# A banded attention and MoE kernel: limits on ScalarE's queue, a shorter flag, values loaded ahead, bias tables in three column parts, identity products on TensorE

## The reference

```python
q, k, v: (2, 8, 768, 64);  n_global = 8;  n_local = 96
scores = (1 / sqrt(64)) * q @ k.T
rel = pos[:, None] - pos[None, :]
is_global = pos[None, :] < n_global
is_local = (rel >= 0) & (rel < n_local)
dist = where(is_global & ~is_local, n_local, abs(rel))
scores += -slopes[head] * dist                 # slopes = 2 ** (-(head + 1)), 8 heads
scores = where(is_global | is_local, scores, -1e9)
attn_out = softmax(scores) @ v
x = attn_out, as 1536 rows of 512
x = rmsnorm(x) * rms_g;  x = (silu(x @ w_gate) * (x @ w_val)) @ w_out
out = sum over the top 2 of 8 experts of weight * (relu(x @ w1[e]) @ w2[e])
```

## Time and profile before

| | |
|---|---|
| Median of 3 runs | 792.08 us (790.52 to 793.17) |
| The profiled execution | 793.64 us |
| Its span, first to last instruction | 791.9 us |
| TensorE busy | 770.3 us, 97% of the span |
| VectorE, ScalarE, GpSimd busy | 381.7, 321.3, 203.6 us |
| Mean granted clock of TensorE | 0.993 of full speed |

### The profile page before, as it was taken

One profiled execution on the slowest core, in us unless ns is written; L12 is line 12 of the kernel. 1 busy time (PEld: TensorE's weight loads), 2 busy tenths in 40 slices (PEclk: granted clock), 3 DMA queues, 4 the chain that ended last, 5 costly groups with the idle time before them and its releaser, 6 DMA issues.

```text
span 791.9 us, 11494 instructions
## 1 busy us (share of the span) xinstructions
PE 770.3 (97%) x4294; PEld 626.5 (79%) x4294; DVE 381.7 (48%) x723; ACT 321.3 (41%) x627; POOL 203.6 (26%) x273
## 2 busy tenths in 40 slices
PE   6999989999999999999999999999999999999994
PEld 4777667887878887878888987788898889898883
DVE  6777775553624235343245463535264454454331
ACT  4777874441334123351134632434243344443321
POOL 4568750000000300002300145141333423232311
PEclk9999999999999999999999999999999999999997
DMA  7868403510010000100313365336254365645221
GB/s 183 210 151 269 114 18 111 159 55 0 1 54 1 0 1 1 53 1 1 106 54 120 111 180 138 94 86 207 46 175 114 91 190 132 165 153 140 49 46 23
DMA packets 76378, 75.29 MB, mean 95 GB/s; under 512 B 46302, under 2 KB 53982, under 8 KB 76320
## 3 DMA queue, kind: packets, MB, share of 16 engines
q1 hardware_dynamic: 68560, 61.64, 26.4%
q0 software_dynamic: 7760, 12.89, 8.2%
HBM read 62.32 MB, written 13.75 MB: 96 GB/s over the span
## 4 chain that ended last, share of the span: by engine, by line
PE 92%; DVE 4%; issue 2%; ACT 1%; POOL 1%; DVEq 0%; POOLq 0%; ACTq 0%
PE banks L515 26%; PE banks L546 13%; PE banks L1048 11%; PE banks L1069 10%; PE banks L1111 8%; PE banks L1077 4%; PE banks L1090 4%; PE banks L1687 3%; PE banks L1722 3%; PE banks L1702 2%; PE banks L1657 2%; PE banks L1683 1%; PE banks L1039 1%; PE banks L1025 1%; PE banks L1086 1%
## 5 line engine op out<-in xcount | busy, mean ns | idle before, releaser
L515 PE MATMUL banks<-XN,W_mid 128*128 128x512 f32 x552 | 134.5, 396 | 0.0
L515 PEld LDWEIGHTS banks<-XN,W_mid 128*128 128x128 f32 x552 | 103.5, 188 | 25.5 <-issue 1.0
L406 POOL DMA_INDIRECT slots<-entry,slot_x x24 | 24.5, 1019 | 268.1 <-DVE slot_x L837 261.7
L1069 PE MATMUL banks<-W_mid,XN 128*128 128x512 f32 x240 | 72.2, 399 | 0.0
L515 PE MATMUL banks<-XN,W 128*128 128x512 f32 x288 | 70.5, 397 | 0.0
L515 PEld LDWEIGHTS banks<-XN,W 128*128 128x128 f32 x288 | 53.5, 188 | 14.3 <-issue 2.0
L652 ACT ACTIVATE HT<-act_b 128x512 fp32r<-128x512 f32 x36 | 22.8, 634 | 95.3 <-DVE act_b L758 87.2
L1602 POOL TENSOR_TENSOR prob<-prob,rinv 128x512 f32<-128x512 f32 (+1 forms) x47 | 46.8, 996 | 40.4 <-DVE rinv L1895 40.3
L1111 PE MATMUL banks<-W_mid,XN 128*128 128x512 f32 x180 | 56.6, 406 | 0.0
L756 DVE TENSOR_TENSOR act_b<-act_b,banks 128x512 f32<-128x512 f32 x36 | 24.7, 685 | 64.1 <-ACT act_b L645 56.8
L936 POOL DMA_INDIRECT out_dram<-xT x16 | 27.7, 1729 | 103.5 <-DVE xT L1250 98.2
(11 more groups left out here) (232 smaller groups left out, 1437.2 us busy)
## 6 DMA issues: line engine op xcount, KB each, us to landing
stage<-in_moe_w_dram SPq DMA_DIRECT2D x64, 512.0 KB
rawv<-in_v_dram SPq DMA_DIRECT2D x16, 192.0 KB, 3.1
out_dram<-zrow SPq DMA_DIRECT2D x1, 3072.0 KB, 12.6
moe_rows<-xT SPq DMA_DIRECT2D x12, 256.0 KB, 2.5
rawq<-in_q_dram SPq DMA_DIRECT2D x14, 192.0 KB, 3.1
rawk<-in_k_dram SPq DMA_DIRECT2D x14, 192.0 KB, 3.3
stage<-in_moe_w_gate_dram SPq DMA_DIRECT2D x4, 512.0 KB
stage<-in_moe_w_val_dram SPq DMA_DIRECT2D x4, 512.0 KB
```

Of the source, the lines that this page charges most:

```text
L515: last = nc.tensor.matmul(bank[2 * kind + n % 2][:], up_weight(kind, hw, k, c), xn[:, hx, k, :], start=(m == 0 and k == 0), stop=(m == 2 a ...
L1069: last = nc.tensor.matmul(bank[5 + t][:], he_pair[:, k, hh, t * P:(t + 1) * P], w2_part(e, hw, k), start=(q == 1), stop=(q == 24))
```

## The change

The two limits are loaded from ScalarE's queue, ahead of its table load, and no longer from SyncE's. SyncE loads the values of pair 0 right after the first halves of queries and keys, and makes the shifted values of pair 0 ahead of the loads of pair 1. VectorE reaches the flag by four operations behind the limits where there were six, all of the form with one scalar and two inputs. The tables are made in three column parts (128, 256, 256) with a semaphore for each, so that score 0, 1 and 2 wait for a part each. TensorE multiplies the identity by itself nine times ahead of the flag and twice ahead of score 0; nobody reads the result (bank 4). Preparations 2 and 3 of pair 0 stand behind score 2 in TensorE's order and behind the exponentials of unit 1 in ScalarE's, and each preparation of pair 1 is given one unit later (`prep_round`).

```diff
@@ sync
-            sp.dma_start(lims_i[:, 0, :], n_global.bitcast(I32).partition_broadcast(P)).then_inc(s_lim, 16)
-            sp.dma_start(lims_i[:, 1, :], n_local.bitcast(I32).partition_broadcast(P)).then_inc(s_lim, 16)
...
+            load_values(0)
             load_queries_keys(0)
-            load_values(0)
             for m in range(PAIRS):
+                if m == 0:
+                    shifted_values(m)
                 if m + 1 < PAIRS:
                     load_queries_keys(m + 1)
                 if m >= 1:
                     load_values(m)
-                shifted_values(m)
+                    shifted_values(m)
...
+        def prep_round(w):
+            return w % QT - (1 if w < QT else 0)
+        def has_prep(w):
+            return w // QT + 1 < PAIRS and 0 <= prep_round(w) < ROUNDS
...
-            return bank[7 - r if m == 0 else 7]
+            return bank[7 - r % 2 if m == 0 else 7]
@@ tensor
+            def idle_products(count):
+                for n in range(count):
+                    nc.tensor.matmul(bank[4][:, 0:P], ident[:], ident[:], start=True, stop=True)
+
+            idle_products(9)
             def prep(m, r):
                 if m >= 1:
                     pe.wait_ge(s_prepA, ROUNDS * m + r)
+                elif r >= 2:
+                    pe.wait_ge(s_prepA, r - 1)
...
                 if w == 1:
+                    pe.wait_ge(s_bias_next, 2)
+                if w == 2:
                     pe.wait_ge(s_bias, 2)
...
-                for r in range(3):
+                for r in range(2):
                     prep(0, r)
+                idle_products(2)
                 score(0)
-                prep(0, 3)
                 score(1)
                 score(2)
+                for r in range(2, ROUNDS):
+                    prep(0, r)
@@ scalar
+            act.dma_start(lims_i[:, 0, :], n_global.bitcast(I32).partition_broadcast(P)).then_inc(s_lim, 16)
+            act.dma_start(lims_i[:, 1, :], n_local.bitcast(I32).partition_broadcast(P)).then_inc(s_lim, 16)
             nc.scalar.preload_act_table_set("natural_log_exp_and_others")
...
+                first_far_bias(slice(0, P), 1, s_bias_first)
                 prep(0, 0)
                 prep(0, 1)
-                prep(0, 2)
-                far_bias(1, slice(P, BW))
-                prep(0, 3)
+                first_far_bias(slice(P, P + CW), 2, s_bias_next)
+                first_far_bias(slice(P + CW, BW), 3, s_bias)
                 expo(0)
                 expo(1)
+                prep(0, 2)
+                prep(0, 3)
@@ vector
-            link(nc.vector.tensor_scalar(dist, rel, 0.0, float(FAR), ALU.is_lt, ALU.mult))
+            link(nc.vector.scalar_tensor_tensor(out=dist, in0=rel, scalar=0.0, in1=rel, op0=ALU.is_lt, op1=ALU.mult))
             dve.wait_ge(s_lim, 32)
-            link(nc.vector.tensor_copy(lims[:], lims_i[:, :, 0].bitcast(U32)))
-            link(nc.vector.scalar_tensor_tensor(out=lims[:], in0=lims_i[:, :, 1], scalar=4294967296.0, in1=lims[:],
-                                                op0=ALU.mult, op1=ALU.add))
+            link(nc.vector.scalar_tensor_tensor(out=lims[:], in0=lims_i[:, :, 1], scalar=4294967296.0,
+                                                in1=lims_i[:, :, 0].bitcast(U32), op0=ALU.mult, op1=ALU.add))
...
-            link(nc.vector.tensor_scalar(fits[:], nG, float(GW), None, ALU.is_le))
-            link(nc.vector.scalar_tensor_tensor(out=fits[:], in0=nL, scalar=1.0, in1=fits[:], op0=ALU.is_ge, op1=ALU.mult))
-            link(nc.vector.scalar_tensor_tensor(out=fits[:], in0=nL, scalar=float(PW + 1), in1=fits[:], op0=ALU.is_le,
+            link(nc.vector.scalar_tensor_tensor(out=fits[:], in0=nL, scalar=float(PW + 1), in1=nL, op0=ALU.is_le,
+                                                op1=ALU.min))
+            link(nc.vector.scalar_tensor_tensor(out=fits[:], in0=nG, scalar=float(GW), in1=fits[:], op0=ALU.is_le,
                                                 op1=ALU.mult))
-            nc.vector.tensor_copy(banded[:], fits[:]).then_inc(sems["banded"], 1)
+            nc.vector.scalar_tensor_tensor(out=banded[:], in0=fits[:], scalar=0.0, in1=fits[:], op0=ALU.max, op1=ALU.mult)\
+                .then_inc(sems["banded"], 1)
             dve.wait_ge(s_pos, 14)
-            for c, done, tables in ((slice(0, P), 1, s_bias_first), (slice(P, BW), 2, s_bias)):
-                link(nc.vector.tensor_tensor(rel[:, c], rel[:, c], dist[:, c], ALU.add))
+            for c, done, tables in ((slice(0, P), 1, s_bias_first), (slice(P, P + CW), 2, s_bias_next),
+                                    (slice(P + CW, BW), 3, s_bias)):
+                link(nc.vector.scalar_tensor_tensor(out=rel[:, c], in0=dist[:, c], scalar=-float(FAR), in1=rel[:, c],
+                                                    op0=ALU.mult, op1=ALU.add))
```

More of the change, by code:

```diff
@@ L1785, in expo, with far_bias, first_far_bias @@
                         .then_inc(s_exp, 1)
-            def far_bias(h, c=slice(0, BW)):
-                if h == 1:
-                    act.wait_ge(s_dist, 1 if c.stop == P else 2)
-                nc.scalar.activation(bias[:, h, c], dist[:, c], ACT.Copy, scale=-(2.0 ** (-8.0 * (h + 1) / H)))\
-                    .then_inc(s_bias_first if c.stop == P else s_bias, 1)
+            def far_bias(h):
+                nc.scalar.activation(bias[:, h], dist, ACT.Copy, scale=-(2.0 ** (-8.0 * (h + 1) / H))).then_inc(s_bias, 1)
+            def first_far_bias(c, done, tables):
+                act.wait_ge(s_dist, done)
+                nc.scalar.activation(bias[:, 1, c], dist[:, c], ACT.Copy, scale=-(2.0 ** (-16.0 / H))).then_inc(tables, 1)
             def out_even(g):
```

11 lines of the change are left out of this document (5 added, 6 removed).

## The result

| kernel | executions | median us | lowest to highest | ratio to before, 95% interval |
|---|---|---|---|---|
| before | 22 | 793.46 | 790.52 to 795.24 | 1 |
| changed | 22 | 795.20 | 793.33 to 796.85 | 1.0022 [1.0015, 1.0029] |

The changed kernel is slower by 0.22%, 1.74 us. The sign and the size are near the forecast's (1.3 us slower, "within 0.3%"), but the time itself lies 1.9 us above the 793.3 forecast and on the upper edge of the range. The profiled execution took 795.15 us, its span 793.2, with a granted clock of 0.991 over the whole span (before: 793.64, 791.9 and 0.993).

A forecast was written before the change was run, and what follows sets the result against it. TensorE was taken to bound the kernel (92% of the chain); third score 13.16 + 12.65 + 0.96 + 0.1 = 26.87 against 25.60 at unit 5, 1.3 us slower, median 793.3, range 791.0 to 795.2.

The forecast's parts named there:

- The flag ... 1.34 earlier: VectorE's path to the flag: limits land at 4.01, four operations follow, tables begin at 4.67, 1.34 us earlier.
- Tables ... 1.20 more: VectorE's tables in three parts take 6.01 us instead of 4.81, 1.20 more, with 0.07 a part for the new form.
- contention 0.35: VectorE's tables lose 0.35 us while GpSimd still fills its constants (bounds 0 and 1.05), ending at 11.03.
- From the tables to score 2: Tables end at 11.03 instead of 10.82, first maximum at 11.30, so the third score starts at 13.16 instead of 12.95.
- A wait of 2 us or more: TensorE ahead of score 2: idle about 2 us at the slow clock, 3 at the fast, where before 0.65.
- Moved preparations + 0.96: TensorE between the third score and unit 5: two preparations now stand there, adding 2 x 0.48 = 0.96 us.
- allowance 0.1: Score 3's wait for ScalarE's copy of the last transposes: 0.1 us at the slow clock, 0.4 at the fast.
- The slow stretch then holds as much work as the one before did: TensorE's clock from about score 2: as much slow work as before, no difference; bounds 1.36 us less or more.
- the clock comes back one stretch later: Rival, chance 0.17: slow stretch begins at score 2 and holds twice the work, 1.36 us more; 2.7 slower, 794.8.
- The base: The kernel before: 792.08 us median of the runs shown, the profiled execution 1.56 above it; expected median 793.3.
- The fall at 104 us: Lower clock after TensorE's 1.25 us wait at 104.42; rival that it doesn't recur, chance 0.08, worth 1.7 us.
- Loads: SyncE's loads leave about 4 us later; pair 3's keys land at 40.6 against need at 41.7, hidden.

The follow-up runs named there:

- e7: The changed kernel with the two limits back at the head of SyncE's queue; 794.40 us, ratio 1.0026 to the kernel before.
- e5: The kernel before with the moved preparations alone (pair 0's 2 and 3 behind score 2, pair 1's one unit later); 794.31 us, ratio 1.0018.
- e8: From e2: limits on SyncE's queue, eight products ahead of the flag, unit 0's maximum and exponentials ahead of the third table part; 794.50 us, ratio 1.0015.
- e9: e8 with SyncE's order wholly as before the change, pair 1's queries and keys ahead of pair 0's shifted values; 790.60 us, ratio 0.9967.
- e3: The changed kernel with eight more identity products between scores 1 and 2; 793.82 us, ratio 1.0013 to the kernel before.
- e6: The changed kernel with the tables in two column parts (128 and 512) instead of three; 794.02 us, ratio 1.0005 to the kernel before.
- e1: The changed kernel without its eleven identity products; 795.52 us, ratio 1.0031 to the kernel before.
- e11: e9 without any identity product; 793.46 us, ratio 0.9999 to the kernel before.
- e2: The changed kernel with preparations 2 and 3 of pair 0 back behind scores 0 and 1; 793.01 us, ratio 0.9997 to the kernel before.

## Why the prediction was right or wrong

**"The flag ... 1.34 earlier": off.** The forecast let the limits land at 4.01. The first operation on them began at 4.37, and the tables at 5.16 instead of 4.67: 0.85 earlier than before. From ScalarE's queue the limits took 2.7 and 3.0 us to land, where I had added only 0.15 to the 2.3 and 2.6 of the earlier trace rows. The four operations themselves took 0.79 to the first table operation, forecast 0.66; the last of them took 0.28 us (0.16 in e7), and the tables stood behind it. The comparison over 640 columns took 0.83, forecast 0.8, and hid.

**"Tables ... 1.20 more": nearly right, "contention 0.35": wrong.** From 5.16 to 10.98 the tables took 5.82 us, 1.01 more than before, where 6.01 + 0.35 = 6.36 was forecast. The new form of the first operation cost nothing (0.28 us at 5.16, the addition's time) where 0.07 a part was allowed. The scalar operation that ran while GpSimd filled its constants took 0.29 (at 5.47), no more than before. The port rule of the Trainium skill (SBUF — State Buffer, "Who interferes with whom") that I weighed lets such an operation be blocked while GpSimd holds the shared ports; in e7, where it began at 4.91 instead, it took 0.39, so it lost 0.1 us there and nothing here. This error and that of the flag cancel, and the tables end at 10.98, forecast 11.03.

**From the tables to score 2: 0.45 us too long.** Score 2 came at 12.80, not at 13.16. The forecast carried over the 1.86 us that lay between the first maximum (11.09) and score 2 (12.95); after, there were 1.41 (11.39 to 12.80). In the kernel before it was not the exponentials that came last, but score 1, whose products fill TensorE from 11.80 up to score 2. e5 shows it: the exponentials of unit 0 began 0.26 us earlier there (11.55 instead of 11.81), and score 2 still came at 12.95. The tables did hold score 2, but by way of score 1, which starts when its own table is ready (11.07 in e5) and ran at the lower level. After the split only the exponentials were left to wait for.

**"A wait of 2 us or more" ahead of score 2: right** (2.60), and e8 and e9 bear out the reason given: with the first maximum ahead of the third part score 2 came at 11.52 and 11.68. About 0.4 of the 1.1 to 1.3 us is the earlier flag, which e7 had too (12.34); the rest is the order. The doubt whether the transposes between the products and score 0 would keep the fast level was not borne out: scores 0 and 1 ran fast.

**"Moved preparations + 0.96": right in kind, the size between two.** The 0.48 us of the chain overlap with what follows. From start to start two preparations take 0.71 us at the upper level (13.98 to 14.69 in e3) and 1.33 at the lower (14.65 to 15.98 in the changed kernel). e5 measured 1.2 us for the move alone. The copy that score 3 waits for cost 0.15 in the changed kernel (allowance 0.1) and 0.41 where the clock held (allowance 0.4).

**"The slow stretch then holds as much work as the one before did": this step failed.** That was a term of 0, with bounds of 1.36 either way. Before, the slow stretch behind the start of score 2 ended near 15.5. I priced it at 1.36, but the 0.87 us of a fast score in the earlier trace rows is only the chain's part of it. From start to start a slow score takes 1.89 us (12.95 to 14.84) and a fast one 1.04 (12.94 to 13.98 in e3), three transposes 0.69 (14.84 to 15.53) and 0.38: 1.16 us in all. After, the stretch lasted to 18.4, and e3 prices it at 2.4. The term that I put at 0 was thus about 1.2 us. With 0.71 for the preparations and the wait of 0.15 it makes, within 0.1 us, the 14.74 us from score 2 to unit 5, where there were 12.58 before and the forecast had 13.71. In mechanism this is the rival "the clock comes back one stretch later", to which I gave 0.17. My error was to take the length of the stretch from the kernel before, where TensorE had been slow since its first instruction, and to apply it to one where the clock falls anew. Nor does the slow stretch begin at score 2, as that rival has it: it began 1.25 us ahead of it in the changed kernel and 1.6 behind it in e7.

**The base was 1.4 us too low.** Three executions of the kernel before had a median of 792.08; over 22 it is 793.46. With that base the forecast's own +1.3 us would have read 794.8. This alone is three quarters of the 1.9 us. The error is in the sum's last line: the profiled execution stood 1.56 above the three runs' median, and I read that as its peculiarity, where it stood near the middle of the larger set.

**The fall at 104 us.** I used as evidence that a wait of 1.25 us drops the clock, and gave 0.08 to its absence. The same instruction waits 1.25 or 1.26 us in the profiles of all thirteen kernels of this study, and in two of them alone (before and e6) was it slow behind that wait. It was a chance event of one execution, and a poor witness for the wait of 2.60.

**Loads:** those of pair 3 stayed hidden, as forecast: the key loads were issued from 36.74 us on instead of 32.73, and the transposes at 42.48 did not wait. The load order mattered once preparations were early again (e8 against e9, 3.9 us by the medians, 3.8 by the ratios), which the forecast had not considered.

**Still open.** Whether the limits landed 0.4 us later for ScalarE's queue or for the query loads that travel at the same time: e7 moves both. Why the clock falls in a given wait in some executions and not in others: no run here tells. The 22 executions of the changed kernel fall in two groups, 8 at 793.3 to 794.0 (mean granted clock 0.993 to 0.994) and 14 at 795.0 to 796.9 (0.988 to 0.991); that these differ by the slow stretch after 12.8 us is argued from e3, not shown. How typical the profile of the kernel before is: its execution had the fall at 104 us and a mean granted clock of 0.993, while 68 of its 84 executions beside the experiments record 0.995 or more. They are only 0.6 to 0.8 us quicker than the others by the medians, where the fall at 104 us costs 1.4. So the profiled execution may have begun quicker than most, and 25.53 be too early a mark; no run shows it.

## What to carry to other kernels

A split that lets the first piece start earlier helps only if its consumer's next instruction does not stand behind all pieces: look at what the queue does after the piece (here the maximum behind the third part), and move that first. Work that has filled a wait is not free to move: behind the wait it costs its full time, and at the lower clock nearly twice that. When the effect is a few tenths of a per cent, three executions are no base, and a single clock fall in one profile is no rule.

## What the runs showed of the hardware

- Products on identity tiles ahead of the work bring TensorE to its upper level earlier: three transposes took 0.54 us behind them (5.98) against 0.89 without (e1, at 6.08). The moment differs from profile to profile: in e3, e7 and e8 those transposes were still slow (0.90, 0.85 and 0.89), and TensorE was fast from score 0 on. The products were worth 2.5 to 2.9 us where the waits behind them were at most 1.33 us (e9 against e11) and nothing that the runs can tell where one of 2.60 us followed (changed against e1).
- The falls of the clock seen at the beginning and at 104 to 107 us came around a wait of 1.25 us or more, but need not begin inside it. The fall began within the wait in the changed kernel (11.55, wait to 12.80) and in e2 (12.65), and after TensorE had resumed in the kernel before (104.6, resumed at 104.42), in e9 (12.45, resumed at 11.68) and in e7 (13.9, resumed at 12.34). What the slow stretch costs depends on how much work lies in it: 5.35 us in the changed kernel, 6.55 in e7.
- In the first microseconds of these profiles the recorded clock can't be trusted: e1's window from 12.79 to 18.50 reads 1.00, though its rows have the durations of the changed kernel's, where the record reads 0.51. In the changed kernel, where TensorE's rows had become fast before, the record shows the fall; in e1, where they never had, it doesn't. Here is e1's window, with the columns as above:

```profile
12.79:18.50 5.71, 5.56 (x20) 3.54 (x20) 1.15 (x5) 3.28 (x11) 1.66 (x2) 1.00 0.25 58
```

- The clock can fall and return within a few microseconds of nearly full work. In e9 TensorE waited 1.33 us, and behind it was busy for 3.77 of 3.82 us at a mean granted clock of 0.60:

```profile
11.68:15.50 3.82, 3.77 (x15) 2.09 (x16) 1.65 (x7) 2.66 (x9) 1.65 (x2) 0.60 1.13 262
```

- VectorE's first operation on the two limits took 1.20 us as a cast and 0.16 as a form with two tensor inputs, on the same two elements. In e7 that form began at 3.93, at the moment of the old cast (3.94), and took 0.16 too, with GpSimd filling its constants both times: the kind of operation is what matters, not the moment.
